# Three-stage token mixer on one core: unit slots, two output buffers, early first operands, parts of the token loads, padded tails

## The reference

```python
# attention without scores
q_s = softmax of q over the 64 values;  k_s = softmax of k over the 576 tokens
attn = einsum(q_s, einsum(k_s, v))              # x: [8, 576, 512]
# token mixing and the first channel mixing (hidden width 1536)
h  = np.maximum(x.T @ w_tok1, 0.0) @ w_tok2;    u = x + h.T
x2 = u + np.maximum(u @ w_ch1, 0.0) @ w_ch2
# second channel mixing (hidden width 2048) on a layer norm
xn = (x2 - mean) / np.sqrt(var + 1e-06) * g_ln
out = x2 + np.maximum(xn @ moe2_w_ch1, 0.0) @ moe2_w_ch2
```

## Time and profile before

| | |
|---|---|
| Median of 3 runs | 1726.64 us (1726.27 to 1731.54) |
| The profiled execution | 1728.29 us, of which 1726.5 us from first to last instruction |
| PE busy | 1532.1 us, 89% |
| DVE, ACT, POOL busy | 1086.4, 697.5, 299.6 us |
| Mean granted TensorE clock | 0.953 of full speed |
| DMA | 429.27 MB, mean 249 GB/s |

### The profile page before, as it was taken

How to read it: one execution, slowest core, us unless ns; L and a number is a source line. 1 busy time by engine, 2 the same in 40 slices (tenths; PEclk the granted TensorE clock), 3 DMA queues, 4 the chain that set the end, 5 groups by cost and what they waited for, 6 DMA issues and landing times.

```text
span 1726.5 us, 19768 instructions
## 1 busy us (share of the span) xinstructions
PE 1532.1 (89%) x7584; PEld 1357.6 (79%) x7584; DVE 1086.4 (63%) x1167; ACT 697.5 (40%) x844; POOL 299.6 (17%) x309
## 2 busy tenths in 40 slices
PE   6999997689789688779899989998999899899999
PEld 5888886578678577668789878887888788788888
DVE  7878865474476278267469577566746665774266
ACT  5555554342343253253344343244334434432332
POOL 5677763311321313210000000000000000000000
PEclk9999999889899899989999999999999999999999
DMA  7888868768868868966857756864776577567656
GB/s 239 265 274 259 278 232 317 301 205 307 315 234 319 330 242 310 355 242 202 288 181 243 278 179 197 285 235 163 233 284 208 168 246 265 169 217 248 241 186 202
DMA packets 149373, 429.27 MB, mean 249 GB/s; under 512 B 13280, under 2 KB 42528, under 8 KB 149280
## 3 DMA queue, kind: packets, MB, share of 16 engines
q1 hardware_dynamic: 131808, 361.94, 61.8%
q0 software_dynamic: 17472, 66.07, 10.5%
HBM read 348.26 MB, written 79.69 MB: 248 GB/s over the span
## 4 chain that ended last, share of the span: by engine, by line
PE 62%; DMA 14%; DVE 12%; ACT 7%; issue 4%; POOL 1%; SPq 1%; DVEq 0%; ACTq 0%; POOLq 0%
PE ps L1082 20%; PE ps L1083 19%; PE ps L1084 19%; DMA w_scratch_C<-w_out 5%; DMA w_scratch_B<-w_out 3%; DMA w_ring<-w_scratch_B 3%; ACT w_out L519 2%; DMA xn<-y_scratch 2%; DVE x_lo L790 2%; DVE q_den L725 1%; ACT x_hi L535 1%; DVE w_out L796 1%; DVE o_lo L935 1%; DMA w_ring<-w_scratch_C 1%; POOL q_lo L440 1%
## 5 line engine op out<-in xcount | busy, mean ns | idle before, releaser
L1082 PE MATMUL ps<-x_hi,w_ring 128*128 128x462 f32 (+1 forms) x980 | 376.9, 385 | 90.2 <-ACT h L618 49.5
L1082 PE MATMUL ps<-o_hi,w_ring 128*128 128x462 f32 (+1 forms) x980 | 374.6, 382 | 67.0 <-DVE o_lo L935 60.2
L640 ACT CAST o_hi<-h 128x924 fp32r<-128x924 f32 (+1 forms) x245 | 234.2, 963 | 361.1 <-PE ps L1084 342.3
L1083 PE MATMUL ps<-x_lo,w_ring 128*128 128x462 f32 (+1 forms) x980 | 373.8, 381 | 0.0
L1084 PE MATMUL ps<-x_hi,w_ring 128*128 128x462 f32 (+1 forms) x980 | 372.9, 380 | 0.0
L1083 PE MATMUL ps<-o_lo,w_ring 128*128 128x462 f32 (+1 forms) x980 | 372.3, 380 | 0.0
L1084 PE MATMUL ps<-o_hi,w_ring 128*128 128x462 f32 (+1 forms) x980 | 371.9, 379 | 0.0
L935 DVE TENSOR_TENSOR o_lo<-h,o_hi 128x924 fp32r<-128x924 f32 (+1 forms) x245 | 275.9, 1130 | 140.9 <-ACT o_hi L640 140.8
L1082 PEld LDWEIGHTS ps<-x_hi,w_ring 128*128 128x128 f32 x980 | 190.3, 194 | 124.5 <-ACT h L618 53.4
L1082 PEld LDWEIGHTS ps<-o_hi,w_ring 128*128 128x128 f32 x980 | 190.8, 195 | 94.5 <-issue 65.9
L905 DVE TENSOR_TENSOR h<-ps,h 128x924 f32<-128x924 f32 (+1 forms) x105 | 117.2, 1116 | 165.0 <-PE ps L1084 164.9
(11 more groups left out here) (122 smaller groups left out, 1703.9 us busy)
## 6 DMA issues: line engine op xcount, KB each, us to landing
w_ring<-w_scratch_C SPq DMA_DIRECT2D x280, 512.0 KB, 3.5
w_ring<-w_scratch_B SPq DMA_DIRECT2D x210, 512.0 KB, 4.8
w_scratch_C<-w_out POOLq DMA_DIRECT2D x16, 1792.0 KB, 11.5
w_scratch_B<-w_out POOLq DMA_DIRECT2D x12, 1792.0 KB, 7.2
kt<-kT SPq DMA_DIRECT2D x32, 288.0 KB, 5.7
u_scratch<-u_out SPq DMA_DIRECT2D x32, 288.0 KB, 2.5
qt<-q SPq DMA_DIRECT2D x32, 256.0 KB, 4.3
ke<-k SPq DMA_DIRECT2D x32, 256.0 KB, 4.6
```

The source lines that it names most:

```text
L640: nc.scalar.copy(o_hi[:, g % RO, :, 0:c.n], src).then_inc(o_hi_made, 1)
L1082: mm(dst, a_hi, b_hi, start=start, stop=False, skip_group_check=onto)
L1083: mm(dst, a_hi, b_lo, start=False, stop=False, skip_group_check=onto)
```

## The change

- **Units.** Two output buffers: the second lies in `last_pair`, memory that the last pair of hidden blocks of stage C uses later. `hi_unit(n)` waits for the store of unit n-2. Eight units are made in stage A. The others have fixed slots, counted in entries from the start of stage B: four at entries 1, 6, 11 and 16, sixteen at entries 22, 31, 40 up to 157. DVE makes the low part in the two slots behind. In stage A POOL sums a unit where it made the low part before, makes the low part at the end of the step, and ACT's `hi_unit` moves to the end of the step too.
- **First operands of the second half.** `hi_o` and `lo_o` of its first two entries (in C three) are issued in the last mixing-in call. The last two of the seven `x` pairs move from that call to the mixing-out call.
- **Tokens.** `load_x` and `load_res` are four DMAs of a quarter each, put one by one between ring loads: `x` in the mixing-out call before, `res` in the second and third calls. The store of the last quarter moves behind the ring load of the next call. The first `x` is loaded ahead of the first ring entries and waits for two batches instead of four, and `sum_x(0, 0)` is issued on DVE early in the last batch.
- **Tails.** The unused 64 rows of the tail chunks are set to zero or hold the low part, and all tail matmuls and transposes take 128 rows.
- **Squares** of the layer norm are split over two products.

The diff, cut to its core:

```diff
-    CONSTS = 6
+    CONSTS = 10
+    UNITS_A = NB
+    HI_AT = {1 + 5 * i: UNITS_A + i for i in range(U0["C"] - UNITS_A)}
+    HI_AT.update({22 + 9 * i: U0["C"] + i for i in range(UNITS["C"])})
...
+        w_out = (w_out0, last_pair[:, 0:14 * 2 * P].bitcast(f32r).rearrange("p (q s f) -> p q s f", q=7, s=2))
+        def units_stored(eng, n):
+            eng.wait_ge(wp_stored[0], 16 * ((n + 1) // 2))
+            eng.wait_ge(wp_stored[1], 16 * (n // 2))
...
 @block.sync
+            def load_x(pos, c):
+                if c == 0 and pos >= NSG:
+                    sp.wait_ge(y_stored, 64 * (pos - NSG + 1))
+                if c == 0 and pos > 0:
+                    sp.wait_ge(x_lo_made, 7 * pos)
+                sp.dma_start(xn[:, c * n:(c + 1) * n], tokens(source["BC"[pos // NSG]], pos % NSG)[:, c, :])\
+                  .then_inc(x_in, 16)
...
+            sp.wait_ge(u_stored, 16 * NC * 2)
+            for c in range(NC):
+                load_x(0, c)
             for n in range(RW):
                 load_entry(n)
-            sp.wait_ge(u_stored, 16 * NC * 4)
-            load_x(0)
             step(NB - 1, 0)
+            phase_a_over(sp)
             for c in CALLS:
-                if c.j == 0 and c.pos + 1 < NX:
-                    load_x(c.pos + 1)
-                if c.j == 1:
-                    if c.index == 1:
-                        phase_a_over(sp)
-                    load_res(c)
...
+                for n in range(7 * c.epp):
+                    p, e = n // c.epp, n % c.epp
+                    if c.e0 + n + RW < ALL_ENTRIES:
+                        load_entry(c.e0 + n + RW)
+                    if c.pos == 0 and c.j == 0 and p in (0, 2, 4, 6):
+                        load_x(1, p // 2)
+                    if c.j in (1, 2) and p in (1, 4):
+                        load_res(c.pos, 2 * c.j - 2 + p // 4)
+                    if c.j < 0 and c.pos + 2 < NX and c.pos != NSG - 1 and p in (2, 3, 4, 5) and e == 0:
+                        load_x(c.pos + 2, p - 2)
...
+                    if c.j == 0 and c.pos > 0 and p == 1:
+                        store(CALLS[c.index - 1], 6, 1, 0)
 @block.gpsimd, step of stage A
                 load_unit(i)
                 if later:
                     sub_q(i + 1, ST)
+                sum_unit(i - 1)
+                if later:
+                    lo_q(i + 1)
                 lo_unit(i - 1)
                 store_unit(i - 1)
-                if later:
-                    lo_q(i + 1)
-                if i < NB - 1:
-                    sum_unit(i)
 @block.scalar
             def hi_unit(n):
                 act.wait_ge(wp_sum, 4 * (n + 1))
-                wait(act, wp_stored, 16 * n)
-                nc.scalar.copy(w_out[:, :, 0, :], w_op[:, n % 2, 0:7, :]).then_inc(wp_hi, 1)
+                wait(act, wp_stored[n % 2], 16 * (n // 2))
+                nc.scalar.copy(w_out[n % 2][:, :, 0, :], w_op[:, n % 2, 0:7, :]).then_inc(wp_hi, 1)
...
-                if not first:
-                    hi_unit(i - 1)
                 for m in range(ND):
                     act.wait_ge(r_done, ND * i + m + 1)
...
                 if later:
                     hi_q(i + 1, ST[3:])
+                if later and not first:
+                    hi_unit(i - 1)
...
+                        if c.e0 + p in HI_AT:
+                            hi_unit(HI_AT[c.e0 + p])
+                        if last and p < 5 and c.pos + 1 < NX and c.pos != NSG - 1:
                             hi_x(c.pos + 1, p)
+                        if last and p == 3:
+                            hi_o(CALLS[c.index + 1], 0, 0)
+                        if last and p == 5:
+                            hi_o(CALLS[c.index + 1], 0, 1)
+                        if last and p == 6 and CALLS[c.index + 1].epp > 3:
+                            hi_o(CALLS[c.index + 1], 0, 2)
 @block.vector
                     norm_kv(i)
+                    if later == 0:
+                        sum_x(0, 0)
                     dve.wait_ge(u_done, 2 * NC * i)
...
+                        if last and split and p == 4:
+                            lo_x(c.pos + 1, 2)
+                            lo_x(c.pos + 1, 3)
+                        if last and p == 5:
+                            lo_o(after, 0, 0)
+                            lo_o(after, 0, 1)
 @block.tensor
-                        x = mm(dst, ke[0:rows, t, c * P:(c + 1) * P], vt[0:rows, t, c, :],
+                        x = mm(dst, ke[:, t, c * P:(c + 1) * P], vt[:, t, c, :],
...
-                mm(dst, q_hi[0:rows, t, cols], t1_lo[0:rows, t, :], start=False, stop=False)
-                return mm(dst, q_hi[0:2 * rows, t, cols], t1_hi[0:2 * rows, t, :], start=False, stop=True)
+                mm(dst, q_hi[:, t, cols], t1_lo[:, t, :], start=False, stop=False)
+                return mm(dst, q_hi[:, t, cols], t1_hi[:, t, :], start=False, stop=True)
```

231 lines of the change are left out of this document (121 added, 110 removed).

## The result

| | before | after |
|---|---|---|
| Median | 1726.45 us (4 runs, 1724.38 to 1731.54) | 1595.75 us (4 runs, 1592.24 to 1598.32) |
| Ratio, 95% interval | | 0.9238 (0.9207 to 0.9268) |
| The profiled execution | 1728.29 us | 1593.26 us, span 1591.5 us |
| Mean granted clock | 0.953 | 0.981 |

The change saves 130.7 us (7.6%). The forecast was 1544 us; the time lies inside the range, 52 us above the point, outside the 1525 to 1568 us of the forecast proper and next to the value of the first rival.

What follows compares the result with a forecast made beforehand. PE was taken as the engine everything serves, idle in gaps, with DMA next. Savings of 17 (stage A), 19.5, 77, 11.5 (stage B) and 58.4 (C) sum to 183.4 us, giving 1544 us, range 1512 to 1600.

Steps and rivals of the forecast that it cites:

- first rival: DMA engines become the bound of stage B and stage A stays at 30 us: 1600 us, chance 0.17.
- the wait of the last batch: Stage A, last batch: `sum_x(0, 0)` waits for `xn` on DVE ahead of `lo_qT`; priced 0 to 8 us, 6 taken.
- the period: Stage A: distance from batch to batch falls from 31.0 to 27.8 us (26.3 to 30).
- B0, first half: Stage B, first position: two buffers end ACT's waits; 74 us (66 to 84), 19.5 less.
- Second half: Second half of stage B's first position: receives three units, 19.8 MB at 360 GB/s; left at 55 us.
- direct wait for unit 11: B0, second half: its third entry needs unit 11, whose ring load lands about 8 us late.
- B1 to B3: Stage B: large gaps go, DMA is left; 342 us, 77 less, including 22 us of late loads and low parts.
- Stage C: 714.5 us, 58.4 less than 772.9, DMA no bound, a position at about 143.5 us.
- third rival: Split operands come late because DVE is full in the last call; ten transitions keep 3 us: 1586 us, chance 0.13.
- Transitions of stage B: First half to second half: DVE is late next; 0.8 us at each of ten transitions in place of some 8.
- B4: Last position of stage B, no unit left in it: 107 us, 11.5 less.
- the slower rival: Quarter loads choke SP's ring, 80 loads of 462 KB replacing 20: 1742 us, slower than before, chance 0.02.

Runs made afterwards that it cites:

- e1: The changed kernel with `sum_x(0, 0)` moved back on DVE behind the low parts `lo_qT` and `r_lo` in stage A's last batch: 1580.79 us, ratio 0.9145.
- v1: e1 with the rest of the last batch's extra work on DVE and ACT moved behind the copies of `u_out`: 1578.48 us, ratio 0.9115.
- e2: The changed kernel with tail matmuls and transposes of 64 rows again: 1601.72 us, ratio 0.9273.
- e8: e1 with three quarters of v and, from the third batch, of k transposed not loaded in stage A: 1580.37 us, ratio 0.9125.
- e6: The changed kernel storing only one of seven products of each stage C unit, the other operands left out: 1567.50 us, ratio 0.9055.
- e7: The changed kernel with DVE making only an eighth of the low part of each stage C unit: 1578.34 us, ratio 0.9111.
- v2: v1 with the sixteen slots of stage C's units moved out of the last mixing-in call and first mixing-out entries: 1569.55 us, ratio 0.9073.
- e4: The changed kernel with the second half's first operands made after the mixing-in calls again, all seven x pairs inside the last call: 1641.98 us, ratio 0.9499.
- e3: The changed kernel with tokens (`xn`, `res`) loaded whole at their old places and the last store where it was: 1633.93 us, ratio 0.9466.
- v3: v1 with x pairs of the mixing-out call spread out or made later, token loads later to match: 1580.86 us, ratio 0.9125.

## Why the prediction was right, and where it was not

The range held, the forecast proper (1525 to 1568 us) did not. Five of the six stretches came out longer than forecast, so the errors didn't cancel each other; the time is inside because the range was drawn out to the first rival's 1600.

**Stage A, the wait of the last batch: mis-sized.** The step was there, with its place, its queue and its witness (DVE waiting for `xn`, forecast about 6 us, measured 7.16). Priced at 6 us within bounds of 0 to 8, it cost 10.2 us in the batch itself and 12.5 at the start of stage B (e1 against after; 2.1 of the 12.5 lie in the six batches before, which are alike in both). DVE was held for the wait and for its sum of 2.32 us. PE stood for 7.97 us of that, inside the bounds, and then worked 5.5 us at a clock of 0.52, which is some 2.6 us more. The prediction had priced this slow clock for the gaps that it removed, and not for the one that it added.

**Stage A, the end of the last batch: left out.** It takes 5.6 us more than before, with one wait of 3.16 us for a copy of `u_out` behind DVE's new work. The sum had no term for it. v1, which puts this work and ACT's behind the copies, takes all of it back, but the whole gains nothing from that.

**Stage A, the period: 28.5 us, forecast 27.8.** The tails freed PE for 2.2 us, and 0.8 to 1.1 of them reached the period (e2): the size of the term (2.7) was near, and adding it in full was not right. `q_den` gave more than the 1.2 us that was taken: it lasts 1.16 us in place of 3.38. DVE and POOL around it:

```profile
212.44 0.74 POOL L421 TENSOR_TENSOR w_op<-w_op 128x256 f32<-128x256 f32 x1
213.15 0.74 POOL L423 TENSOR_TENSOR w_op<-w_op 128x256 f32<-128x256 f32 x1
213.96 0.74 POOL L425 TENSOR_TENSOR w_op<-w_op 128x256 f32<-128x256 f32 x1
```
```profile
212.75 1.16 DVE L768 TENSOR_SCALAR q_den<-q_sum 128x16 f32<-128x16 f32 x1
```

PE's part and DVE's part thus measured 2.2 us each, and the period fell by 2.5. Of the limits that the text had named as near, the DMA rate is excluded by e8, though the share stands at 0.92 in the batch above. PE has 2.4 us of slack. The chain of waits goes from the tail of q, which lands after 7 us in place of 4.1, over its sums, `q_den` and POOL's `q_lo` to PE; which link sets the 28 us stays open.

**B0, first half: the number right, in part by luck.** 75.9 us for 74, at 339 GB/s, the lower of the two full rates of the earlier trace rows. But it moved 25.7 MB (75.9 x 339) where 27.7 were counted, and of PE's 15.6 idle us 5.23 stand in its second product, which begins when DVE's last copy of `u_out` is done (4.90 before). **Second half: too low by 6.8.** It moved 20.3 MB (61.8 x 328), near the 19.8 counted, so the count was right and the rate of 360 GB/s was not reached. Whether the rate is the cause isn't shown: e6, with less stored, gives 58.9, and e7, with all of it, 59.2. One stall of 2.95 us stands where the direct wait for unit 11 was expected (8 us late by the sum), one of 2.73 us for a ring load follows later, and one of 2.35 us for `o_lo` stands at the transition. The prediction had worked out that stall and yet left this half at its 55 us.

**B1 to B3: the two limits right, their size wrong.** 363.2 for 342. The entries alone are 317.4, and the term of 22 + 2.4 us for late loads and low parts measured 46. Of them 21 to 25 come from the stored bytes (e6) and 8 to 13 come from DVE's low parts (e7, v2). The prediction had argued that a demand of 366 GB/s lies inside the two full rates. The stretch ran at 317 with waits, at a DMA share of 0.88 where about 0.95 was forecast: here such a demand was not met without them. The first rival said 375, so B1 to B3 ended between the two; of the rival's other parts B0 did not go its way, and stage A did by its time (13.4 us over) but by another cause, the last batch.

**Stage C: right.** A position of 143.4 us was forecast at 143.5, the clock at 1.00, no wait of PE for tokens or ring loads. The third rival, split operands that come late, did not happen here: the wait at a transition is 0.37 us. e4 shows that the step carries the gain: without it C takes 38.0 us more. e3 shows the other half, 21.5 us. Together 59.5, where C gained 59.7 us.

**Transitions of stage B: in part the third rival.** The waits for `o_lo` at the transitions of B0, B1 and B4 are 2.35, 4.22 and 1.14 us, where 0.8 was taken, and the waits for `o_lo` over the whole kernel are 22.9 us, where about 10 were forecast (60.2 before). e4 and v2 show where they come from: DVE is full around the end of the first halves.

**B4: too low by 6.4.** No unit is left in it, and its DMA share is 0.69; the bunched x pairs of the next stage and short waits for `o_lo` had no term in the sum. v3 gets 2.5 of the 6.4.

**The quarter loads do not choke the queue** (the slower rival): the ring loads of C land in 3.8 us, where they took 3.5 before, those of B in 5.5 (4.8 before), and PE waits for none in C.

## What to carry to other kernels

Before an instruction is put early into the queue of an engine, look up what it waits for and who waits for that engine: `sum_x` half a batch early took back most of what seven shorter batches had saved. A gap on PE costs its length plus the slow clock behind it where nothing else is late, an added gap like a removed one. Where other waits lie near, as in B1 to B3, taking it away moves part of it into them; so price a removed stall by what is late next, and a stretch whose demand comes near the full rate by the rate that was seen, not by the demand. Where a buffer is waited for, try a longer, fixed distance between its uses before a second buffer.

## What the runs showed of the hardware

- **DVE and POOL slow each other down, by more than one instruction.** `q_den` starts 0.31 us into POOL's second sum and ends with the third (213.15 + 0.74 = 213.89 us, `q_den` ends at 213.91). The Trainium skill (SBUF — State Buffer, section "Who interferes with whom") blocks the later one until the other's instruction ends, which would have been 213.18; here and in the earlier trace rows it lasted one instruction longer. The same section of the Trainium skill has instructions of DVE with two SBUF inputs contend with POOL's reads, and the trace agrees: `x_lo` 4.46 us for two beside POOL's sums, 2.14 without. The last of POOL's four sums took 1.50 us in place of 0.73 there, so both lose. A DVE instruction with one input in PSUM keeps its time beside the sums (`h<-ps,h` at 332.21 us: 1.11).
- The same in the last batch of stage A, where POOL's two low parts took 5.04 us instead of 4.20, and DVE's instructions 2.5 instead of 1.1:

```profile
247.01 5.04 POOL L431 TENSOR_TENSOR w_out<-w_op,w_out 128x1024 fp32r<-128x1024 f32 x2 [11.08 <-ACT w_out L547]
```
```profile
247.82 2.56 DVE L833 TENSOR_TENSOR x_lo<-xn,x_hi 128x924 fp32r<-128x924 f32 x1 [0.72 <-ACT x_hi L563]
250.49 2.53 DVE L819 TENSOR_TENSOR xn<-xn 128x924 f32<-128x924 f32 x1
```

- **A small load can land later than a large one.** The tail of q (128 KB into 64 partitions) lands in 6.9 to 7.7 us (medians) in the changed kernels, the loads of 256 KB ahead of it in 3.9 to 4.5, and with less traffic it stays so (e8). In the kernel before it took 4.1. What in the new order delays it wasn't found.
- **A gap costs by what lies around it.** The same transition without early operands costs 7.6 us in stage C and 3 to 4 in B1 to B3, where 9 us of short waits go at the same time (e4).
- **The slow clock follows a wait of 8 us too.** Behind the 7.97 us in the last batch of stage A PE's clock is 0.52 over 5.5 us, and matmuls of 256 columns start 0.21 us apart in place of 0.12.
